# Transposed probabilities in two PSUM banks by turns instead of one, in the first batch's attention

## The chip, the cores and the metric

The kernel runs on one core of a Trainium2 chip, in one launch. The metric is the device time in microseconds, the median of several runs. All tensors are float32.

## What is computed

Three layers follow each other, on a batch of 4 sequences of 768 tokens with 8 heads of 40 channels (320 in all).

1. A recurrence over the tokens with a 40 x 40 state for each head: `state = state * w - (state a) b^T + v k^T`, read by `r`.
2. A mixture of four attention experts, of which the gate picks two for each token. This is the part around the change:

```python
for e in range(E):                       # E = 4 experts, head width 64
    q, k, v = x @ wq[e], x @ wk[e], x @ wv[e]
    scores = np.where(causal, -1e9, scale * (q @ k.transpose(0, 2, 1)))
    a = np.exp(scores - scores.max(-1, keepdims=True))
    a /= a.sum(-1, keepdims=True) + 1e-09
    ye = a @ v @ wo[e]
    out += mask_e * w_e * ye             # gate of the expert for the token
```

3. A gated MLP with 1,024 channels whose second half is normalised and mixed over the tokens by a 768 x 768 matrix (`w_spatial`), multiplied by the first half and projected by `w_out`.

## The kernel before, in words

The recurrence (lines 27 to 1026) takes the first half of the time; its last outputs land in memory, and layers 2 and 3 (`experts_and_mlp`, lines 1027 to 1633) follow batch by batch. Each engine has a program of its own, written out by hand, and they are tied by semaphores: `then_inc` on the producer, `wait_ge` ahead of the consumer. An engine carries out its program in order, so an instruction that waits holds up everything behind it.

TensorE's program for layers 2 and 3 is the loop of lines 1463 to 1484. For batch n it turns the tokens (`turn_x`), multiplies out values, gates, queries and keys, and goes through the attention in 15 steps. Between the steps' parts it issues slices of the *dense* work of batch n-1, that is the mixing over tokens (L1440) and the output projection (L1452). The function `slot` hands them out evenly. Batch 0 has no batch before it, so its attention runs without such slices.

**A step.** The attention of a batch has 12 units (`STEPS`): 6 blocks of 128 queries times 2 pairs of experts. Unit s has block i = s // 2 and pair s % 2, and is causal, so its scores have i + 1 blocks of 128 keys for each of the pair's two experts. At step s TensorE works on three units at once:

- `scores(n, s)` (L1362): scores of unit s into banks 0 to 3;
- `turn(n, m)` (L1382) for each piece m of the step: the probabilities of unit s-2 are transposed, up to four blocks of 128 x 128 at a time, into one PSUM bank, `T_BANK` = 4;
- `times_v(n, s-3)` (L1394): the values times the transposed probabilities of unit s-3, into bank 5.

**Pieces.** The list `pieces` (lines 1114 to 1120) is fixed: unit s-2 has 2 (i' + 1) blocks, for i' its own query block, cut into pieces of four and a last one of two where that is left. In even steps from 4 on a *share* piece of two blocks follows, which transposes each expert's gate over its sum. A batch has 30 pieces. Step by step from 2 to 14 their numbers are 1, 1, 2, 1, 3, 2, 3, 2, 4, 3, 4, 3 and 1.

**The other engines.** VectorE takes the maximum of unit s from the scores' banks and writes the masked scores to `probs` (`maxima`, L1535), makes the shares (L1543 to L1549), and multiplies the product with the values by the transposed share (`scaled_o`, L1557). ScalarE's program in a step alternates (lines 1288 to 1297): copy of the step's first piece out of its bank (`turned`, L1228 is the copying helper), exponential of unit s for the first expert (L1242), copy of the second piece, exponential for the second expert, then the copies of the third and fourth piece.

**Who waits for whom.** `p_turned` counts the transposed pieces and `p_read` the copied ones. Piece m of `turn` waits for `p_read` of piece m-1 (line 1374), since all pieces share bank 4. `times_v` waits for the copies of the pieces of the step before. Behind the 15 steps of batch 0 come `turn_x(1)` and `values_and_gates(1)` (54 transpositions and matmuls), and then `hidden(0)` (L1409), which writes banks 6 and 7 (`M_BANK` = 6 and the next). For batch 0 nothing in layers 2 and 3 uses bank 6 before `hidden(0)`.

The lines that matter:

```python
if n > 0 or m > 0:
    pe.wait_ge(p_read, at(n, p_read, m))           # turn, lines 1373, 1374
...
copy(dst.rearrange("p j t -> p (j t)"), bank[T_BANK][:, 0:k * P]).then_inc(p_read, 1)   # turned, line 1235
```

Of the kernel before, what the change touches and what calls it, by code (L numbers as in the profile page):

```python
# [10 lines left out]
P = 128  # L11
# [1015 lines left out]
def experts_and_mlp(nc, z, x_dram, weights, out_dram, shared):  # L1027
# [15 lines left out]
    ident, hide, before = shared.ident, shared.hide, shared.before  # L1043
    w_qk, w_vg, w_oi, x_tok = shared.w_qk, shared.w_vg, shared.w_oi, shared.x_tok

    with ExitStack() as ctx:
# [5 lines left out]
        def sem(name, count, first=0):  # L1052

            s = shared.stack.enter_context(nc.semaphore(name))
            per[s] = count
            start[s] = first
            return s

        def at(n, s, c):

            return n * per[s] + (c + start[s])
# [26 lines left out]
        out_tok = sb("out_tok", [P, BLOCKS, F])  # L1088


        banks = shared.banks
        bank = [banks[:, i, :] for i in range(8)]
        T_BANK, O_BANK, M_BANK = 4, 5, 6
# [27 lines left out]
        PIECES = len(pieces)  # L1121
        p_turned = sem("p_turned", PIECES)
        p_read = sem("p_read", PIECES)
# [25 lines left out]
        def pieces_of(s):  # L1149

            return [m for m, piece in enumerate(pieces) if piece[0] == s]

        def probs_upto(s):


            return max(m for m, piece in enumerate(pieces) if piece[0] <= s + 2 and piece[1] == "probs") + 1
# [11 lines left out]
        def dense_upto(n, s, k):  # L1168

            return DENSE * (slots.index((s, k)) + 1) // len(slots) if n else 0  # L1170

        def dense_from(n, s, k):

            i = slots.index((s, k))
            return dense_upto(n, *slots[i - 1]) if i else 0

        def groups_of(n, lo, hi):


            ends = [BLOCKS * (g + 1) for g in range(2 * DT)] + [SPATIAL + DT * (g + 1) for g in range(BLOCKS)]  # L1180
            return [g for g, end in enumerate(ends) if lo < end <= hi]
# [11 lines left out]
        def after_recurrence(engine):  # L1193


            for done, count in shared.recurrence_done:
                engine.wait_ge(done, count)
# [27 lines left out]
        @block.scalar  # L1225
        def _(act):
            def copy(dst, src):
                return act.activation(dst, src, ACT.Copy)  # L1228

            def turned(n, m):  # L1230

                s, what, j, k = pieces[m]
                act.wait_ge(p_turned, at(n, p_turned, m + 1))
                dst = probs_t[:, s % 2, j:j + k, :] if what == "probs" else share_t[:, j % 2, :, :]
                copy(dst.rearrange("p j t -> p (j t)"), bank[T_BANK][:, 0:k * P]).then_inc(p_read, 1)

            def exponentials(n, s, a):

                i, e = s // EP, 2 * (s % EP) + a
                width = (i + 1) * P  # L1240
                act.wait_ge(s_read, at(n, s_read, 2 * s + a + 1))
                act.activation(probs[:, s % 3, a, 0:width], probs[:, s % 3, a, 0:width], ACT.Exp, scale=-1.0,  # L1242
                               bias=neg_max[:, i, e:e + 1], accum_out=den[:, i, e:e + 1]).then_inc(probs_ready, 1)

            def outputs(n, lo, hi):

                m = n - 1
                for g in groups_of(n, lo, hi):
                    if n > 0 and g >= 2 * DT:
                        i = g - 2 * DT  # L1250
                        act.wait_ge(y_ready2, at(m, y_ready2, i + 1))
                        if m > 0:
                            act.wait_ge(y_stored, at(m - 1, y_stored, 16 * BLOCKS))
                        copy(out_tok[:, i, :], bank[M_BANK + i % 2][:, 0:F]).then_inc(y_read, 1)

            after_recurrence(act)
            for n in range(B + 1):
                m = n - 1
                if n < B:
                    for i in range(1, BLOCKS, 2):  # L1260
                        act.wait_ge(x_turned, at(n, x_turned, i + 1))
                        t = slice(i * P, i * P + P)
                        src = bank[i % 4]
                        copy(x_t[:, 0:2, t], src[:, 0:2 * P].rearrange("p (k t) -> p k t", k=2))
                        copy(shared.x_last[0:LAST, t], src[0:LAST, 2 * P:3 * P]).then_inc(x_read_act, 1)
                if n > 0:
                    for i in range(BLOCKS):
                        act.wait_ge(h_ready, at(m, h_ready, i + 1))
                        act.activation(v_raw[:, i, :], bank[M_BANK + i % 2][:, :], ACT.Relu,
                                       accum_out=stat[:, 0, i:i + 1]).then_inc(h_read, 1)  # L1270
                    act.wait_ge(mean_ready, at(m, mean_ready, 1))
                    for i in range(BLOCKS):
                        act.activation(v_n[:, i, :], v_raw[:, i, :], ACT.Square, bias=stat[:, 1, i:i + 1],
                                       accum_out=stat[:, 2, i:i + 1]).then_inc(squares_ready, 1)
                if n < B:
                    act.wait_ge(gate_step, at(n, gate_step, 7))
                    act.activation(gate[:, 2, :, :], gate[:, 1, :, :], ACT.Exp).then_inc(gate_exp, 1)
                if n > 0:
                    act.wait_ge(norm_step, at(m, norm_step, 1))
                    act.activation(stat[:, 4, :], stat[:, 3, :], ACT.Sqrt).then_inc(root_ready, 1)  # L1280
                if n < B:
                    for j in range(4):
                        act.wait_ge(qk_ready, at(n, qk_ready, j + 1))
                        act.activation(q_t[:, j // 2, (j % 2) * TH:(j % 2) * TH + TH], bank[j][:, 0:TH],
                                       ACT.Copy, scale=float(HD) ** -0.5).then_inc(q_read, 1)

                    outputs(n, 0, dense_upto(n, -1, 0))
                    for s in range(STEPS + 3):
                        outputs(n, dense_from(n, s, 0), dense_upto(n, s, 0))
                        last = len(pieces_of(s)) + 1  # L1290
                        for k in range(max(2, last)):
                            if k + 1 < last:
                                turned(n, pieces_of(s)[k])
                            if k < 2 and s < STEPS:
                                exponentials(n, s, k)
                            if k + 1 <= last:
                                outputs(n, dense_from(n, s, k + 1), dense_upto(n, s, k + 1))
                else:
                    outputs(n, 0, DENSE)

        @block.tensor
        def _(pe):
# [63 lines left out]
            def turn(n, m):  # L1366

                s, what, j, k = pieces[m]
                if what == "probs":
                    pe.wait_ge(probs_ready, at(n, probs_ready, 2 * (s - 1)))  # L1370
                else:
                    pe.wait_ge(share_ready, at(n, share_ready, j + 1))
                if n > 0 or m > 0:
                    pe.wait_ge(p_read, at(n, p_read, m))
                width = (s - 2) // EP + 1
                for x in range(k):
                    if what == "probs":
                        a, c = (j + x) // width, (j + x) % width
                        src = probs[:, (s - 2) % 3, a, c * P:c * P + P]
                    else:  # L1380
                        src = share_b[:, 2 * x:2 * x + 2, :].rearrange("p e d -> p (e d)")
                    ins = pe.transpose(bank[T_BANK][:, x * P:x * P + P], src, ident[:, :])  # L1382
                ins.then_inc(p_turned, 1)

            def times_v(n, s):
# [13 lines left out]
            def hidden(m):  # L1399

                for i in range(BLOCKS):
                    if i < 2:
                        if m > 0:
                            pe.wait_ge(y_read, at(m - 1, y_read, BLOCKS - 1 + i))
                    else:
                        pe.wait_ge(h_read, at(m, h_read, i - 1))
                    pe.wait_ge(o_read, at(m, o_read, i + 1))
                    for q in range(EP):
                        ins = pe.matmul(bank[M_BANK + i % 2][:, :], o_t[:, q, i * P:i * P + P], w_oi[:, q, DH:],  # L1409
                                        start=(q == 0), stop=(q == EP - 1))  # L1410
                    ins.then_inc(h_ready, 1)
# [362 lines left out]
```

## Time and profile before

| | |
|---|---|
| median of 3 timed runs | 1078.49 us (1078.14 to 1078.82) |
| profiled execution | 1071.31 us, span 1069.5 us |
| mean granted TensorE clock | 0.984 of full speed |
| TensorE busy with matmuls | 989.7 us (93%) |
| VectorE, ScalarE, GpSimd busy | 523.9, 451.9 and 249.2 us |
| first batch's attention | 545.3 to 599.0 us of the span |

The profile shows one execution, and its own time is 7.2 us below the median of the timed runs. Busy times of different engines overlap; for each engine busy time and idle time add up to the span. PE is TensorE's matmuls, PEld its weight loads, DVE is VectorE, ACT is ScalarE. A view of the waits names for each idle time the instruction that ended it. The chain of waits is followed back from the last instruction of the stretch, so its pieces follow each other without overlap.

### The profile page before, as it was taken

Reading aid. Unit: us, or ns where it says so; the run is one execution under the profiler, and the core shown is the slowest. Engines: PE = TensorE matmul, PEld = TensorE weight load, DVE = VectorE, ACT = ScalarE, POOL = GpSimd, SP = SyncE. Lnnn points to the kernel's source line nnn. Section 1 sums busy time; section 2 is a strip of 40 time slices with the busy share of each in tenths; the row PEclk is TensorE's granted clock in tenths of the full one; section 3 lists DMA queues with packets and bytes.
Section 4 is the critical chain, followed back from the end, with each engine's and each line's share of the span. In section 5 each row is a group of like instructions: output and inputs, shape, how many; then the busy total and the mean of one; then the engine's idle time right before and its main releaser. Section 6 shows DMA issues by size and latency. Waiting matters only on the chain.

```text
span 1069.5 us, 36916 instructions
## 1 busy us (share of the span) xinstructions
PE 989.7 (93%) x15696; PEld 708.6 (66%) x15696; DVE 523.9 (49%) x1443; ACT 451.9 (42%) x1116; POOL 249.2 (23%) x352
## 2 busy tenths in 40 slices
PE   1889999999999999998887999999999999999988
PEld 0478888888888888886644654557545665456555
DVE  5357777777777877755343233322433224331220
ACT  1245555655556565553145243442333423434400
POOL 7334454344444534411000001100011000110011
PEclk9869999999999999999999999999999999999989
DMA  5124434334343433221140100001000000000001
GB/s 154 50 67 119 112 110 124 97 100 151 101 124 101 124 95 111 79 70 48 39 164 1 37 1 1 1 19 56 0 1 1 26 13 0 1 1 26 13 0 37
DMA packets 50645, 63.49 MB, mean 59 GB/s; under 512 B 26545, under 2 KB 36593, under 8 KB 50481
## 3 DMA queue, kind: packets, MB, share of 16 engines
q1 hardware_dynamic: 50480, 61.13, 19.6%
q8 instruction: 125, 2.05, 0.8%
q14 instruction: 40, 0.32, 0.1%
HBM read 53.22 MB, written 7.86 MB: 57 GB/s over the span
## 4 chain that ended last, share of the span: by engine, by line
PE 81%; DVE 9%; issue 4%; ACT 3%; POOL 1%; DMA 1%; SPq 1%; DVEq 0%; POOLq 0%; ACTq 0%
PE banks L1440 13%; PE banks L590 10%; PE banks L635 6%; PE banks L1343 6%; PE banks L1382 5%; PE banks L1362 4%; PE banks L1394 4%; PE banks L1422 4%; PE banks L1409 4%; PE banks L1452 4%; PE banks L820 3%; DVE state_z L1016 3%; PE banks L810 3%; PE banks L1329 3%; PE banks L682 2%
## 5 line engine op out<-in xcount | busy, mean ns | idle before, releaser
L473 ACT ACTIVATE powers_z<-powers,parity 128x256 f32<-128x256 f32 x240 | 108.6, 500 | 168.8 <-DVE powers L891 168.8
L1440 PE MATMUL banks<-w_st,v_n 128*128 128x384 f32 x384 | 151.5, 510 | 4.9 <-issue 4.9
L1223 POOL TENSOR_TENSOR v_st<-v_st,u_t 128x384 f32<-128x384 f32 x32 | 31.9, 998 | 513.5 <-DVE v_st L1589 513.5
L635 PE MATMUL banks<-pq,powers_z 64*64 64x64 f32 (+1 forms) x3072 | 135.0, 226 | 6.1 <-ACT pq L465 3.3
L635 PEld LDWEIGHTS banks<-pq,powers_z 64*64 64x64 f32 x3072 | 114.2, 140 | 11.2 <-ACT powers_z L473 4.1
L1228 ACT ACTIVATE probs_t<-banks 128x512 f32<-128x512 f32 (+1 forms) x96 | 52.0, 542 | 145.4 <-PE banks L1382 145.4
L434 POOL TENSOR_TENSOR state<-state_sum,dc 128x160 f32<-128x160 f32 x92 | 68.6, 746 | 177.7 <-DVE state_sum L1002 177.5
L1440 PEld LDWEIGHTS banks<-w_st,v_n 128*128 128x128 f32 x384 | 65.5, 194 | 44.1 <-issue 19.9
L994 DVE SCALAR_TENSOR_TENSOR vu_tok<-banks,minus,vz_tok 128x80 f32<-128x80 f32 x192 | 48.9, 296 | 81.0 <-PE banks L820 80.9
L1535 DVE CUSTOM_DVE_ANT_0 probs<-banks,hide 128x128 f32<-128x128 f32 (+5 forms) x96 | 56.0, 622 | 66.3 <-PE banks L1362 66.1
L1242 ACT ACTIVATE probs<-probs,neg_max 128x128 f32<-128x128 f32 (+5 forms) x96 | 63.2, 660 | 34.5 <-DVE neg_max L1535 34.5
L395 POOL TENSOR_TENSOR kb_ch<-kb_raw,s_ch 128x512 f32<-128x512 f32 x48 | 60.5, 1282 | 52.0 <-issue 33.6
L1382 PEld LDWEIGHTS banks<-ident,probs 128*128 128x128 f32 x336 | 39.1, 141 | 45.9 <-issue 35.0
L1382 PE MATMUL banks<-ident,probs 128*128 128x128 f32 x336 | 54.0, 277 | 13.1 <-ACT probs_t L1228 11.5
L1452 PE MATMUL banks<-w,v_st 128*128 128x320 f32 x192 | 62.1, 443 | 0.0
L1557 DVE TENSOR_TENSOR o_t<-banks,share_t 128x256 f32<-128x256 f32 x24 | 10.2, 425 | 97.4 <-PE banks L1394 96.1
L1589 DVE TENSOR_TENSOR v_st<-banks,bias 128x384 f32<-128x384 f32 x32 | 17.8, 556 | 75.5 <-PE banks L1440 75.3
L601 PE MATMUL banks<-az_ch,kb_ch 128*32 128x64 f32 x1536 | 31.9, 225 | 24.6 <-ACT az_ch L465 23.6
L590 PE MATMUL banks<-ident,state_z 128*128 128x128 f32 x384 | 52.4, 280 | 0.8 <-ACT vu_ch L465 0.8
L1362 PE MATMUL banks<-k_t,q_t 64*128 64x512 f32 (+3 forms) x256 | 48.9, 481 | 1.4 <-DVE k_t L1620 0.7
L1394 PEld LDWEIGHTS banks<-probs_t,vg 128*64 128x64 f32 x672 | 36.6, 139 | 20.5 <-issue 11.3
L1394 PE MATMUL banks<-probs_t,vg 128*64 128x128 f32 x672 | 48.4, 284 | 0.0
(158 smaller groups left out, 1860.1 us busy)
## 6 DMA issues: line engine op xcount, KB each, us to landing
w_ch<-decays_dram SPq DMA_DIRECT2D x48, 160.0 KB
kb_raw<-kb_ch_dram SPq DMA_DIRECT2D x48, 160.0 KB
vz_tok<-vz_tok_dram SPq DMA_DIRECT2D x24, 320.0 KB, 3.5
r_all<-rz_ch_dram SPq DMA_DIRECT2D x48, 160.0 KB
x_dram<-y_tok SPq DMA_DIRECT2D x384, 10.0 KB, 1.9
a_raw<-a_ch_dram SPq DMA_DIRECT2D x48, 80.0 KB
vc_tok<-vc_tok_dram SPq DMA_DIRECT2D x24, 160.0 KB, 3.8
r_all<-r_ch_dram SPq DMA_DIRECT2D x48, 80.0 KB
```

The source lines that it names most:

```text
L395: pool.tensor_tensor(kb_ch[:, u % 3, a * W:a * W + W].rearrange("p (k s t) -> p k s t", s=2, t=C), kb_raw[:, u % 2, a * W:a * W + W].rearr ...
L434: pool.tensor_tensor(state[:, d % 2], state_sum[:, :, :], dc[:, v % 4, d].unsqueeze(2).to_broadcast([P, Q, D]), ALU.mult)\
L473: act.activation(powers_z[:, i, :, j, :], powers[:, i, :, :], ACT.Copy, scale=parity[:, j:j + 1])\
L590: return pe.transpose(to, src, ident[:, :])
L635: ins = pe.matmul(to[r, k * n:k * n + n], powers_z[r, i, k, :, :].rearrange("p j t -> p (j t)"), right, start=True, stop=True)
L1242: act.activation(probs[:, s % 3, a, 0:width], probs[:, s % 3, a, 0:width], ACT.Exp, scale=-1.0, bias=neg_max[:, i, e:e + 1], accum_out=den ...
L1343: ins = pe.matmul(bank[j % 4][:, 0:TH], w_qk[:, which, k, q * P:q * P + P], x_of(k, t), start=(k == 0), stop=(k == NK - 1))
L1362: ins = pe.matmul(bank[2 * a + (j if width > 512 else s % 2)][:, 0:w], q_t[rows, p, i * P:i * P + P], k_t[rows, p, c:c + w], start=True, s ...
L1382: ins = pe.transpose(bank[T_BANK][:, x * P:x * P + P], src, ident[:, :])
L1394: ins = pe.matmul(bank[O_BANK][64 * a:64 * a + HD, p * P:p * P + P], vg[:, j, e * HD:e * HD + HD], probs_t[:, s % 2, a * (i + 1) + j, :], ...
L1440: ins = pe.matmul(bank[M_BANK + j % 2][:, 0:TH], v_n[:, i, d * P:d * P + P], w_st[:, i, t], start=(i == 0), stop=(i == BLOCKS - 1))
L1452: ins = pe.matmul(bank[M_BANK + i % 2][:, 0:F], gated[:, d, i * P:i * P + P], w_2[:, d, :], start=(d == 0), stop=(d == DT - 1))
```

## The change

In batch 0 the pieces with an odd number go to bank 6 (`M_BANK`), those with an even number stay in bank 4. The transposition of piece m there waits for the copy of piece m-2 (the semaphore's value m-1) in place of that of piece m-1, and piece 1 waits for none. ScalarE's copy reads the bank of its piece. The first block of `hidden(0)`, which writes bank 6, waits for the copy of batch 0's last piece. For the batches 1 to 3 all stays as it was.

```diff
+        def turn_bank(n, m):
+            return bank[M_BANK if n == 0 and m % 2 else T_BANK]
...
             def turned(n, m):
...
-                copy(dst.rearrange("p j t -> p (j t)"), bank[T_BANK][:, 0:k * P]).then_inc(p_read, 1)
+                copy(dst.rearrange("p j t -> p (j t)"), turn_bank(n, m)[:, 0:k * P]).then_inc(p_read, 1)
...
             def turn(n, m):
...
-                if n > 0 or m > 0:
+                if n > 0:
                     pe.wait_ge(p_read, at(n, p_read, m))
+                elif m > 1:
+                    pe.wait_ge(p_read, at(0, p_read, m - 1))
...
-                    ins = pe.transpose(bank[T_BANK][:, x * P:x * P + P], src, ident[:, :])
+                    ins = pe.transpose(turn_bank(n, m)[:, x * P:x * P + P], src, ident[:, :])
...
             def hidden(m):
                 for i in range(BLOCKS):
                     if i < 2:
                         if m > 0:
                             pe.wait_ge(y_read, at(m - 1, y_read, BLOCKS - 1 + i))
+                        elif i == 0:
+                            pe.wait_ge(p_read, at(0, p_read, PIECES))
```

## Rows read from the trace of the kernel before

**Rows 1.** The page, busy time, share of the span, instructions.

```profile
PE 989.7 (93%) x15696; PEld 708.6 (66%) x15696; DVE 523.9 (49%) x1443; ACT 451.9 (42%) x1116; POOL 249.2 (23%) x352
```

**Rows 2.** Busy time by stage: length, PE, PEld, DVE, ACT, POOL, PEclk, DMA.

```profile
545.30:599.00 53.70, 39.52 (x329) 25.09 (x329) 20.82 (x72) 29.95 (x78) 0.00 (x0) 0.97 0.04 15
599.00:645.00 46.00, 46.00 (x160) 28.57 (x159) 17.46 (x50) 14.94 (x38) 0.00 (x0) 1.00 0.07 22
```

**Rows 3.** Waits of TensorE, 545.3 to 599: total us, times, longest.

```profile
PE banks L1382 <- ACT probs_t L1228: 13.0, 17, 0.8
```

**Rows 4.** Waits of TensorE, from 599 us to the end.

```profile
PE banks L1440 <- issue: 4.9, 1, 4.9
PE banks L1382 <- ACT probs_t L1228: 2.9, 12, 0.2
```

**Rows 5.** Chain of waits, 538 to 600: start, length, what (steps 10, 11, 12).

```profile
572.34 1.49 PE banks L1362 x8
573.83 0.60 PE banks L1382 x4
574.43 0.02 issue
574.45 0.60 ACT probs_t L1228
575.05 0.91 ACT probs L1242 x2
575.96 0.49 ACT probs_t L1228
576.46 0.91 ACT probs L1242 x2
577.37 0.28 ACT probs_t L1228
577.65 0.14 issue
577.79 0.41 PE banks L1382 x2
578.20 1.02 PE banks L1394 x16
...
583.89 1.24 PE banks L1394 x20
...
589.32 0.66 PE banks L1382 x2
589.97 2.33 PE banks L1394 x20
```

**Rows 6.** Groups of VectorE, 545.3 to 599: busy us, mean ns.

```profile
L1535 DVE CUSTOM_DVE_ANT_0 probs<-banks,hide 128x768 f32<-128x768 f32 x4 | 3.7, 955 | 3.2 <-PE banks L1362 3.2
...
L1535 DVE DVE_READ_ACCUMULATOR2_ANT neg_max<- 128x1 f32 x24 | 2.0, 84 | 0.0
```

**Rows 7.** Transpositions and copies, all batches: ns shortest, median, longest.

```profile
L1382 PE MATMUL banks<-ident,probs x336: 272/273/349, 547.8 to 987.1; 128*128 128x128 f32 x168
...
L1228 ACT ACTIVATE probs_t<-banks x96: 363/597/598, 548.4 to 987.4; 128x512 f32<-128x512 f32 x72, 128x256 f32<-128x256 f32 x24
```

**Rows 8.** Busy time around 588 us, columns as in Rows 2.

```profile
586.00:588.00 2.00, 0.72 (x5) 0.54 (x6) 0.00 (x0) 0.95 (x2) 0.00 (x0) 1.00 0.00 0
588.00:590.00 2.00, 1.22 (x8) 0.68 (x10) 0.00 (x0) 0.60 (x1) 0.00 (x0) 0.73 0.00 0
590.00:592.00 2.00, 2.00 (x20) 1.91 (x20) 0.00 (x0) 0.38 (x1) 0.00 (x0) 0.50 0.00 0
```

**Rows 9.** Busy time at the tail, columns as in Rows 2.

```profile
1018.00:1021.00 3.00, 1.35 (x2) 0.84 (x3) 1.55 (x4) 0.00 (x0) 0.00 (x0) 0.66 0.00 0
1021.00:1024.00 3.00, 3.00 (x6) 1.69 (x5) 0.00 (x0) 0.00 (x0) 0.00 (x0) 0.50 0.00 0
```

## The prediction

> **What bounds the kernel now.** I read the page first, then the busy time by stage, the waits of the stage that the change touches, and the chain of waits through it. On the page TensorE is busy for 93% of the span [rows 1], so a change counts only by what it does to TensorE's idle time or to its clock. By stage that share is uneven: in the 53.70 us from 545.3 to 599.0, which is the first batch's attention, TensorE has work for 39.52 us; in the next 46.00 us it has no idle time at all [rows 2]. This stretch is the only place where the change acts, and it is TensorE's alone: what it wins there moves everything behind it forward, because TensorE is the engine that the rest of the program waits for.
>
> The waits say who is late: 17 times, 13.0 us in all, a transposition stands still for ScalarE's copy of the piece before [rows 3]. That is 0.77 us each, and the number fits the code. A piece waits for the copy of the piece before it whenever nothing stands between them in TensorE's program; steps 4 to 13 have 1, 0, 2, 1, 2, 1, 3, 2, 3 and 2 such neighbours (the share piece of an even step included), together 17. Where a piece is the first of its step, the copy had a product with the values and new scores to hide behind, and no wait shows. In the later batches dense matmuls stand between the pieces, and the same kind of wait costs 2.9 us in 12 times, 0.24 us each [rows 4].
>
> The chain through step 10 shows what one such wait is made of [rows 5]: a piece of four blocks takes 0.60 us, 0.02 us later ScalarE copies it for 0.60 us, and 0.14 us after the copy the next piece starts. It also shows ScalarE's own order: copy, exponential, copy, exponential, copy, with 0.91 us for an exponential with its read and 0.49 us from the start of a four-block copy to that of what follows it. That order decides which waits remain.
>
> **Removed.** All 17 waits are for the bank and not for the data: the exponentials that a piece reads are two steps old. With two banks by turns a piece waits for the copy of the piece before last. Removed: 13.0 us [rows 3].
>
> **New waits.** Each is worked out from the durations of [rows 5], with time 0 at the start of the step's first piece. The copy of that piece ends at 0.60 + 0.02 + 0.60 = 1.22, and its bank can be written at 1.36. If the second piece has four blocks TensorE is through with it at 1.21, and a third piece waits 0.15 us; if it has two blocks (0.41 us), at 1.01, and the third waits 0.35 us.
> - Steps 4, 5, 7 and 9 have at most two pieces: nothing.
> - Step 6 (four blocks, two, share): 0.35. Step 8 (four, four, share): 0.15.
> - Step 10 (four, four, two, share): 0.15 for the third. The fourth needs the second's copy, and before that one ScalarE has an exponential to do, which itself waits for VectorE's maximum: it ends about 0.96 + 0.08 us after the scores [rows 6], so the exponential starts at 1.13, the copy at 2.04, it ends at 2.64, and the bank is free at 2.78. TensorE is ready at 1.36 + 0.41 = 1.77: a wait of 1.01 us, the largest.
> - Step 11 (four, four, two): 0.15. Its third copy comes after both exponentials: 2.04 + 0.50 + 0.91 = 3.45, done at 3.82 (0.37 us, as the shortest copies of [rows 7]). No piece of step 11 waits for it, but the second of step 12 does, from 1.77 + 1.24 (values) + 0.60 = 3.61 until 3.96: 0.35.
> - Step 12's share piece: 0.15. Step 13's third piece: 0.15. Step 14: nothing.
>
> The sum is 0.35 + 0.15 + 0.15 + 1.01 + 0.15 + 0.35 + 0.15 + 0.15 = 2.46 us. The waits removed and the waits added make 13.0 - 2.5 = **10.5 us**. The ends for this term: nothing new at all (13.0 us won), or each of the 8 places above waits a full 0.77 us (13.0 - 6.2 = 6.8 us won). I take the worked value: a late copy is the only cost the rows show, and its parts are each seen here.
>
> **Other terms of the edit.** The new wait at the first hidden product stands behind the last copy, which ends at about the time the last product with the values starts; the next batch's 54 transpositions and first matmuls lie between: nothing, and at most 0.14 us if it were not covered. One wait less for piece 1: nothing, TensorE is not stopped there now. TensorE would now write one bank while ScalarE reads another. That happens already in the later batches, beside the dense matmuls, and over all four batches the copies spread no further than 597 to 598 ns from median to longest and the transpositions' median is 273 ns with a shortest of 272 [rows 7]: I take nothing, the median's case. At worst the 50 transpositions of the 17 pieces take the longest row's 349 ns, 50 x 0.076 = 3.8 us more; a gain is excluded by the shortest. VectorE and the DMA queues get no new instruction. VectorE becomes a little tighter, since scores come sooner: in step 10 its two maxima take about 2 us after the scores, while TensorE has 0.6 + 0.6 + 0.15 + 0.41 + 1.0 + 0.41 + 1.0 us until the next scores, so they are not late.
>
> **The clock.** Between 588 and 592 us the granted clock is 0.73 and then 0.50, that is 1.2 GHz in place of 2.4, right after a stretch in which TensorE had 0.72 us of work in 2.00 [rows 8]. The chain prices it: the twenty matmuls with the values that took 1.24 us in step 11 take 2.33 us in step 12, and the share piece before them 0.66 us in place of 0.41 [rows 5]: 1.09 + 0.25 = 1.34 us. In the new order steps 12 and 13 are filled: TensorE idles 0.65 us in some 7 us. I take it that the clock stays up and add **1.3 us**; the ends are 0 and 1.3. The rule that speaks against this is a section of the Trainium skill, TensorE: Matmul & The Clock Gate, "A second HAM failure mode: psum-queue depth-cycling": a kernel whose matmul groups cycle through PSUM banks leaves many very short idle times, and the clock then oscillates. By that rule the result would be the rival with the low clock below; the trace so far speaks otherwise, since its mean over the stretch is 0.97 [rows 2], and the drop at 588 alone makes that up: (2 x 0.27 + 2 x 0.50) / 53.7 = 0.03. Through all the short idle times before it the clock stayed up. At the tail, the idle time of 4.9 us [rows 4] brings the clock down again (0.66 and 0.50 in six microseconds [rows 9]). All this now lies 12 us earlier and may be longer or shorter: a row of 3 us at low clock is worth 3 x (1 - 1.24 / 2.33) = 1.4 us, which I put into the range on both sides.
>
> **Sum.** 10.5 + 1.3 = 11.8 us. The profiled execution took 1071.31 us (span 1069.5); it would take 1059.5. The median of the timed runs is 1078.49 us, 7.2 us more; no view says where that lies, and I take the gain over unchanged: **1066.7 us**.
>
> **Rivals.**
> - *The clock drop stays* somewhere in the stretch, as short as now: 10.5 us won, 1068.0. For: it has already come once here. Against: the gaps around it go. Chance 0.17.
> - *ScalarE becomes the bound.* It has 29.95 us of work in this stretch [rows 2], and would have it in about 42. If its order (copies behind exponentials) delays the transpositions at every one of the 8 places by 0.77 us, 6.8 us plus some of the clock are won: 1071. For: the 1.01 us of step 10 is such a case. Against: 29.95 is well below 42, and TensorE itself is busy 38 of them (39.52 - 1.34). Chance 0.13.
> - *Low clock over the stretch*, the slower one. If the idle times are now cut so finely that the clock stays at 1.2 GHz, its price is 0.47 us for each microsecond that it lasts (1 - 1.24 / 2.33); 22 us of it eat up the 10.5 us. Over the whole stretch TensorE's 38 us of work would be 72, some 19 us more than the stretch has now: 1098. Against: more work in less time than before. Chance 0.02.
> - *The change does not do what it says*, because the waits are for something else or the time won is waited for again at the next stage: 1078.5. Against: the 17 waits name the copy, and the 46.00 us behind the stretch have no idle time [rows 2]. Chance 0.03.
> - My forecast: 0.65.
>
> **How the numbers follow.** 1066.7 is the likeliest case. The range reaches down by 3.5 us (no new waits would give 2.5, the tail's clock 1.4, and both in full are not likely together) and up by 4.3 to the ScalarE case, which takes in the 3.8 us of slower transpositions and the clock drop at 1068.0 with the tail's 1.4: 1063.2 to 1071.0. A measurement of this kernel can tell about 0.2%, 2.2 us, from no change. Every case but two lies beyond that: faster 0.95, same 0.03, slower 0.02.
>
> **What would show it.** Right: the attention stretch is 41 to 43 us long; the 17 waits for the copy become about 8, with 2.5 us in total and a longest of 1.0 in step 10; the clock is 1.00 all through; TensorE's busy time in the stretch is near 38 us; the next stage still takes 46.0 us. Wrong: ScalarE's copies at 0.60 us grown longer (the two banks do collide), transpositions above 273 ns, waits of TensorE for VectorE's maxima, or a granted clock below 1.00 in the stretch.

## The result, and the profile after

The changed kernel took 1059.75 us (median; the kernel before 1078.14 in the same comparison), a ratio of 0.9862 with a 95% interval of 0.9833 to 0.9891: about 14.9 us less. One of its five executions, the profiled one, took 4513 us, with TensorE busy for 4472.8 us on the same 15,696 matmuls that take 982.5 us in the profile below, and a recorded clock of 1.00; it is left out, why it was slow is open, and the profile below is of another run of the same kernel. Three later comparisons of the unchanged pair gave 0.992 (0.9898 to 0.9941), 0.9877 (0.9845 to 0.9908) and 0.9907 (0.9872 to 0.9942). In microseconds the four are 14.9, 8.6, 13.2 and 10.0, in the mean 11.7, against 11.8 forecast. The forecast's gain holds; its absolute 1066.7 us was 7 us too high, and this median lies below the range as a time, while 0.9862 of 1078.49 is 1063.6, inside it. The forecast was counted from a median of three executions, 1078.49, and the 59 executions of the kernel before that came later, on three chips, have medians of 1071.64, 1069.58 and 1069.98.

The length of the attention stretch is the sharper measure, for it repeats to 0.1 us. I take it from the first scores of batch 0 to the first token transposition of batch 1. The busy time by stage, first of the kernel before (profiled again), then of the changed one (columns: length, PE, PEld, DVE, ACT, POOL, PEclk, DMA share, GB/s):

```profile
30.00:85.00 55.00, 44.20 (x966) 33.36 (x964) 31.36 (x76) 25.02 (x58) 22.89 (x28) 0.94 0.26 79
495.00:546.34 51.34, 43.93 (x550) 32.70 (x551) 17.50 (x52) 8.16 (x21) 2.51 (x4) 0.93 0.32 98
546.34:599.21 52.87, 39.43 (x328) 24.96 (x328) 20.27 (x71) 29.92 (x78) 0.00 (x0) 0.97 0.03 12
599.21:1068.50 469.29, 456.13 (x2092) 267.06 (x2090) 141.51 (x420) 155.62 (x398) 31.90 (x32) 1.00 0.04 13
```

```profile
544.79:585.63 40.84, 36.53 (x329) 24.10 (x329) 19.98 (x71) 29.24 (x78) 0.00 (x0) 1.00 0.04 12
585.63:1055.90 470.27, 457.17 (x2092) 267.58 (x2090) 141.53 (x420) 155.73 (x398) 31.96 (x32) 0.99 0.04 13
```

The stretch fell from 52.87 to 40.84 us, 12.03 less; two more profiles of the changed kernel show 40.83 and 40.82. What lies behind it takes the same time as before to 1 us (469.29 and 470.27), so nothing is given back later. The clock is 1.00 all through the stretch. These answer to [rows 2], whose stretch begins 0.72 us earlier, in the wait for the first keys; counted that way the new stretch is 41.6 us, within the 41 to 43 forecast.

The waits of TensorE in the changed kernel (545 to 600 us: total, times, longest), which answer to [rows 3]:

```profile
PE banks L1389 <- ACT probs_t L1233: 3.6, 8, 1.0
PE banks L1367 <- DVE k_t L1629: 0.7, 1, 0.7
PE banks L1367 <- DVE neg_max L1544: 0.7, 2, 0.4
```

Eight waits for a copy are left of seventeen, as many as forecast, but they are worth 3.6 us and not 2.5. In order of time, TensorE's own rows (start, length, what, and in brackets the idle time before it) show each, in steps 6, 8, 10 (twice), 11, 12 (twice) and 13:

```profile
555.00 0.41 PE L1389 MATMUL banks<-ident,share_b 128*128 128x128 f32 x2 [0.56 <-ACT probs_t L1233]
...
561.67 0.41 PE L1389 MATMUL banks<-ident,share_b 128*128 128x128 f32 x2 [0.34 <-ACT probs_t L1233]
...
567.64 1.09 PE L1389 MATMUL banks<-ident,probs 128*128 128x128 f32 x8
569.07 0.41 PE L1389 MATMUL banks<-ident,probs 128*128 128x128 f32 x2 [0.34 <-ACT probs_t L1233]
570.47 0.41 PE L1389 MATMUL banks<-ident,share_b 128*128 128x128 f32 x2 [0.99 <-ACT probs_t L1233]
...
574.76 0.41 PE L1389 MATMUL banks<-ident,probs 128*128 128x128 f32 x2 [0.34 <-ACT probs_t L1233]
...
576.35 0.66 PE L1389 MATMUL banks<-ident,probs 128*128 128x128 f32 x4
577.36 1.11 PE L1389 MATMUL banks<-ident,probs 128*128 128x128 f32 x8 [0.35 <-ACT probs_t L1233]
578.76 0.41 PE L1389 MATMUL banks<-ident,share_b 128*128 128x128 f32 x2 [0.29 <-ACT probs_t L1233]
...
581.78 0.63 PE L1389 MATMUL banks<-ident,probs 128*128 128x128 f32 x4 [0.34 <-ACT probs_t L1233]
```

Why the sizes are off shows in step 9, of which the chain of waits has this row (start, length, what):

```profile
564.17 1.02 PE banks L1389 x8
```

Two pieces of four blocks with no wait between them take 1.02 us, not 0.60 + 0.61: the second adds only 0.42. TensorE's own rows say where the rest is. Four transpositions with a wait behind them take 0.66 us (at 576.35) and eight in a row 1.09 (at 567.64), so four more cost 0.43, 0.11 each, although one lasts 0.27 us [rows 7]: in a row the next starts while the last still runs. Only ahead of a wait does the last one count in full, 0.16 us more. The 0.60 us of [rows 5] is such a piece; it follows the scores at once and has the wait behind it. Without a wait TensorE is through earlier, and waits longer for a copy that comes when it was expected. In step 10 the third piece starts at 569.07, 1.36 us after the first one's place in the chain, 567.71, exactly as forecast.

### The profile page after: what moved, and what is told of

It reads as the page before. It is cut to its first block, busy times and chain, and to the rows that moved or that the text cites. A ratio compares the mean times of both kernels' runs of the same rounds, so it can differ in the third digit from the quotient of the medians.

```text
span 4511.2 us, 36916 instructions
## 1 busy us (share of the span) xinstructions
PE 4472.8 (99%) x15696; PEld 2804.9 (62%) x15696; DVE 534.9 (12%) x1443; ACT 465.9 (10%) x1116; POOL 241.4 (5%) x352
## 4 chain that ended last, share of the span: by engine, by line
PE 99%; POOL 0%; issue 0%; DVE 0%; ACT 0%; DVEq 0%; POOLq 0%; ACTq 0%
PE banks L635 14%; PE banks L590 13%; PE banks L1449 13%; PE banks L1348 8%; PE banks L1461 5%; PE banks L1389 5%; PE banks L1418 5%; PE banks L1431 5%; PE banks L1367 4%; PE banks L1401 4%; PE banks L1334 4%; PE banks L682 3%; PE banks L601 3%; PE banks L820 3%; PE banks L832 3%; PE banks L804 2%
## 5 line engine op out<-in xcount | busy, mean ns | idle before, releaser
L1449 PE MATMUL banks<-w_st,v_n 128*128 128x384 f32 x384 | 597.3, 1762 | 4.9 <-issue 4.9
L635 PE MATMUL banks<-pq,powers_z 64*64 64x64 f32 (+1 forms) x3072 | 564.9, 654 | 0.5 <-ACT d_tok L465 0.5
L635 PEld LDWEIGHTS banks<-pq,powers_z 64*64 64x64 f32 x3072 | 526.9, 597 | 20.0 <-issue 18.4
L590 PE MATMUL banks<-ident,state_z 128*128 128x128 f32 x384 | 258.2, 1016 | 0.0
L1461 PE MATMUL banks<-w,v_st 128*128 128x320 f32 x192 | 244.1, 1490 | 0.0
L1348 PE MATMUL banks<-x_t,w_qk 128*128 128x384 f32 x128 | 240.7, 2153 | 0.0
L590 PEld LDWEIGHTS banks<-ident,state_z 128*128 128x128 f32 x384 | 171.0, 494 | 61.5 <-issue 60.7
L1418 PE MATMUL banks<-w_oi,o_t 128*128 128x512 f32 x96 | 207.1, 2473 | 0.0
L1431 PE MATMUL banks<-o_t,w_oi 128*128 128x384 f32 x128 | 207.1, 1945 | 0.0
L832 PE MATMUL banks<-vu_tok,kb_tok 64*40 64x40 f32 x1536 | 163.9, 406 | 1.4 <-DVE vu_tok L994 1.4
```

The costliest lines, as they stand in the source:

```text
L590: return pe.transpose(to, src, ident[:, :])
L635: ins = pe.matmul(to[r, k * n:k * n + n], powers_z[r, i, k, :, :].rearrange("p j t -> p (j t)"), right, start=True, stop=True)
L832: ins = pe.matmul(bank[S_BANK + q % 2][rows40(x), a * D:a * D + D], kb_tok[rows64(p), u % 3, a, c, x, :], vu_tok[rows64(p), u % 2, c, a, x ...
L1348: ins = pe.matmul(bank[j % 4][:, 0:TH], w_qk[:, which, k, q * P:q * P + P], x_of(k, t), start=(k == 0), stop=(k == NK - 1))
L1431: ins = pe.matmul(bank[M_BANK + j % 2][:, 0:TH], w_oi[:, q, d * P:d * P + P], o_t[:, q, t], start=(q == 0), stop=(q == EP - 1))
L1449: ins = pe.matmul(bank[M_BANK + j % 2][:, 0:TH], v_n[:, i, d * P:d * P + P], w_st[:, i, t], start=(i == 0), stop=(i == BLOCKS - 1))
```

## The experiments

Each comparison ran against the kernel before on the same chip. All stretch lengths are read as above.

### The kernel before and the changed one again

> The kernel before, unchanged, for its own spread and a second profile. Both theories: ratio 1.000 within 0.003; attention of batch 0 is 53.7 us long (52.3 if the clock does not fall in it), 17 waits of 0.77 us. If the profiled and timed executions differ by several us again, the theory that the low-clock time elsewhere (recurrence start and tail) varies from run to run expects that difference there and not in the attention stretch.

> The changed kernel, unchanged. Theory A (waits and local clock only): 10.5 + 1.3 = 11.8 us less than before in the stretch of batch 0's attention, which lasts 41.9 us with 8 waits of 2.5 us in all, longest 1.0; anything beyond 11.8 us in the medians is granted clock outside the stretch. Rival B (more is won inside the stretch): the stretch is 36 to 38 us long. The measured ratio was 0.9862 (about 15 us); A expects 0.989, B 0.984.

Measured: the kernel before against itself 1.0006 (0.9983 to 1.003), stretch 52.87 us, 17 waits of 13.0 us. Its 12 executions ran from 1065.67 to 1079.54 us, so a single time says little here. The changed kernel: 0.992, stretch 40.84 us. The 41.9 us of theory A were counted from 53.70; from 52.87 the same 11.8 us lead to 41.1. So theory A is right about the stretch to 0.3 us, and rival B, more won inside it, is out.

The spread between executions comes in part with the clock: over the 23 executions of the kernel before in this comparison, time and mean granted clock go together with a correlation of -0.86, and 0.001 less clock goes with 0.7 us more; in the two later comparisons the correlation is -0.65, with 0.6 and 0.5 us. Where that lies shows in the traces: most have low-clock microseconds at 35 to 45 us, at 65 to 80 and at 500 to 515, in the recurrence's start and end, some between 50 and 65 too, and together they make from 7 to 31 us. None of these places is touched by the change.

The recorded clock does not account for all of it. The six traces with 13.7 us of low clock in the recurrence reach the first scores between 540.6 and 546.3 us, and the one with the least, 6.8 us, only at 548.6. In that one, the fourth run of the changed kernel, six matmuls of the recurrence take 5.78 us while the recorded clock is 1.00; in the third run they take 3.04 (start, length, what; the row from 34 to 38 us is busy time by stage):

```profile
31.29 5.78 PE L615 MATMUL banks<-r_all,w_ot 128*128 128x512 f32 x6
...
34.00:38.00 4.00, 4.00 (x36) 1.34 (x34) 0.00 (x0) 0.60 (x1) 0.00 (x0) 1.00 0.19 72
```

```profile
29.06 3.04 PE L615 MATMUL banks<-r_all,w_ot 128*128 128x512 f32 x6
```

So a clock of 1.00 has to be read together with durations. In the attention stretch they agree: TensorE's work there is 36.53, 36.53 and 36.52 us in the three traces.

### The banks without the earlier start

```diff
-                if n > 0:
-                    pe.wait_ge(p_read, at(n, p_read, m))
-                elif m > 1:
-                    pe.wait_ge(p_read, at(0, p_read, m - 1))
+                if n > 0 or m > 0:
+                    pe.wait_ge(p_read, at(n, p_read, m))
```

> Two banks by turns, but each piece waits for the copy of the piece before, as before the change. If the gain is the earlier start alone (theory A): ratio 1.000, stretch 53.7 us with 17 waits of 0.77 us. If writing another bank than the one being read is worth something by itself (rival B): a ratio below 0.997 and shorter waits or transpositions.

Measured: ratio 1.0004 (0.9979 to 1.003), stretch 53.08 us, and the waits of the kernel before:

```profile
PE banks L1387 <- ACT probs_t L1233: 13.0, 17, 0.8
```

The second bank alone is worth nothing (its stretch of 53.08 us is 0.2 us longer than before); all of the gain is the wait that it allows to relax.

### Early and late steps alone

```diff
-                    pe.wait_ge(p_read, at(0, p_read, m - 1))
+                    pe.wait_ge(p_read, at(0, p_read, m - 1 if s < 10 else m))    # early; s >= 10 for late
```

(Piece 1 keeps its wait for piece 0 in the version with the late steps.)

> Two banks, but the wait two pieces back only in steps 2 to 9; from step 10 on each piece waits for the copy just before it. Theory A: the stretch is 52.9 - 4.9 = 48.0 us, with the drop of the clock near its end still there; 10 of the old waits of 0.77 us plus 2 new ones; ratio 0.995. Rival C (ScalarE is late in the next steps and takes the early gain back): the stretch is above 50 us.

> The reverse: each piece waits for the copy just before it in steps 2 to 9, two pieces back from step 10 on. Theory A: the stretch is 52.9 - 5.9 = 47.0 us, less 1.3 us more if the drop of the clock goes with the gaps of steps 12 and 13 (45.7 us in all); 7 waits of 0.77 us and 6 new ones; ratio 0.993. If the clock drop has nothing to do with these gaps it stays and the stretch is 47.0 us.

Measured: late only, ratio 0.9933 (0.99 to 0.9965), stretch 45.73 us, the 45.7 of the case in which the clock drop goes; its clock is 1.00 all through. Early only, ratio 0.9954 (0.9924 to 0.9984), 12 waits of 8.7 us, stretch 49.61 us and not 48.0. The difference is a second clock drop. Of the version with the early steps only, the busy time around the two drops:

```profile
574.00:576.00 2.00, 0.63 (x3) 0.46 (x4) 0.00 (x0) 1.63 (x4) 0.00 (x0) 0.90 0.00 0
576.00:578.00 2.00, 2.00 (x18) 1.61 (x17) 0.00 (x0) 0.38 (x1) 0.00 (x0) 0.50 0.00 0
588.00:590.00 2.00, 1.22 (x13) 1.07 (x14) 0.00 (x0) 0.98 (x2) 0.00 (x0) 0.82 0.00 0
590.00:592.00 2.00, 2.00 (x17) 1.67 (x14) 0.50 (x2) 0.00 (x0) 0.00 (x0) 0.50 0.00 0
```

The first follows the three gaps of step 10. Sixteen matmuls with the values take 1.98 us there where the changed kernel has them in 1.09, eight scores 1.92 in place of 1.56, and the share piece 0.66 in place of 0.41: 1.50 us, and 49.61 less that is 48.1. Both drops lie in the half whose waits were kept, none in the filled half. So each half gives what was counted for it; the ratio of 0.9954 is 4.9 us (1.7 to 8.1), as forecast for one drop, but too wide to tell one drop from two.

### Gaps filled, waits kept

```diff
                 ins.then_inc(p_turned, 1)
+                if n == 0 and s >= 10:
+                    for x in range(2):
+                        pe.transpose(bank[M_BANK][:, x * P:x * P + P], ident[:, :], ident[:, :])
```

This is the kernel before with added work whose result nobody reads.

> The kernel before, with one bank and all its waits, and behind each piece from step 10 on two more transpositions of the identity into bank 6, which nobody reads: TensorE has some work in the gaps, no wait goes. Theory A (the clock falls around 588 us because of these gaps, and that is worth 1.34 us): the clock stays at 1.00 through the stretch; 10 of the additions lie in gaps and cost nothing, 5 do not and cost about 0.2 us each, so the stretch is 52.9 - 1.3 + 1.1 = 52.7 us, ratio 1.000. If the clock falls there for another reason: it falls again and the stretch is 54.0 us, ratio 1.001.

Measured: ratio 1.0012 (0.9984 to 1.004), which by itself tells little; the trace tells it. The stretch, and TensorE's work among the gaps of step 12:

```profile
540.55:593.20 52.65, 41.38 (x358) 27.25 (x358) 20.27 (x71) 29.95 (x78) 0.00 (x0) 1.00 0.03 10
580.00:582.00 2.00, 1.44 (x13) 1.20 (x12) 0.00 (x0) 0.60 (x1) 0.00 (x0) 1.00 0.00 0
582.00:584.00 2.00, 1.16 (x9) 0.71 (x7) 0.00 (x0) 1.06 (x2) 0.00 (x0) 1.00 0.00 0
```

The clock stays at 1.00 with all 17 waits in place (10.8 us in all, since the filler takes part of ten of them), and the stretch is 52.65 us against 52.7 expected. So the clock term is about the gaps, and it can be had without removing the waits, though here the filler costs nearly as much as it saves. That is one trace; the kernel before showed the drop in both of its traces and the version with the banks alone in its one.

### ScalarE's order

```diff
-                            if k + 1 < last:
+                            if k + 1 < last and not (n == 0 and k == 1):
                                 turned(n, pieces_of(s)[k])
+                            if n == 0 and k == 0 and last > 2:
+                                turned(n, pieces_of(s)[1])
```

> Two banks as in the change, and in batch 0 ScalarE copies the first two pieces of a step before its two exponentials. Theory A (the wait of 0.99 us in step 10 is the exponential between the two copies): it shrinks to 0.2 to 0.4 us, the others stay, stretch 40.1 us (0.7 less), ratio 0.988. Rival (the wait is ScalarE's total work): the wait moves to the next step and the stretch stays at 40.8 us.

Measured: ratio 0.988 (0.9833 to 0.9927), stretch 39.77 us, 1.07 less than the changed kernel. In step 10 the third piece keeps its wait and the fourth has none:

```profile
572.67 0.41 PE L1391 MATMUL banks<-ident,probs 128*128 128x128 f32 x2 [0.34 <-ACT probs_t L1233]
573.16 0.41 PE L1391 MATMUL banks<-ident,share_b 128*128 128x128 f32 x2
```

The largest remaining wait was the exponential between two copies, as the forecast had it. It was expected to shrink to 0.2 to 0.4 us, for 0.7 us won; it is gone whole, 0.99 us, and TensorE's work is 0.07 us shorter with it. ScalarE carries out the same instructions as before, so their total was not the bound.

### Three banks

```diff
-            return bank[M_BANK if n == 0 and m % 2 else T_BANK]
+            return bank[(T_BANK, M_BANK, M_BANK + 1)[m % 3] if n == 0 else T_BANK]
...
-                elif m > 1:
-                    pe.wait_ge(p_read, at(0, p_read, m - 1))
+                elif m > 2:
+                    pe.wait_ge(p_read, at(0, p_read, m - 2))
```

> Three banks by turns (4, 6, 7) in batch 0, each piece waits for the copy three pieces back. Theory A: nearly all of the 2.5 us of waits left by two banks go, with one of about 0.2 us for VectorE's maxima before the scores of step 8; the stretch is 39.5 us, 2.3 us less than with two banks, ratio 0.987 or lower. If ScalarE's order is the bound (rival C): not more than 0.5 us less than two banks.

Measured: ratio 0.9895 (0.9869 to 0.9921), stretch 37.92 us, 2.92 less than with two banks, where 2.3 were expected: rival C is out. The waits that are left are mostly of another kind (0.38 us of the first row, ahead of the second scores, was there before the change):

```profile
PE banks L1367 <- DVE neg_max L1544: 1.0, 3, 0.4
PE banks L1401 <- DVE o_t L1566: 0.6, 1, 0.6
PE banks L1389 <- ACT probs_t L1233: 0.6, 1, 0.6
```

VectorE is late, and its own row says for whom: it stood still 2.27 us for the share's copy, which ScalarE does behind both exponentials of step 6, and what VectorE has queued behind that product are the maxima that the scores of step 8 wait for:

```profile
556.69 0.43 DVE L1566 TENSOR_TENSOR o_t<-banks,share_t 128x256 f32<-128x256 f32 x1 [2.27 <-ACT share_t L1233]
557.03 0.68 DVE L1544 CUSTOM_DVE_ANT_0 probs<-banks,hide 128x512 f32<-128x512 f32 x1
```

So the last version also puts ScalarE's copies first, and all of them:

```diff
+                            if n == 0:
+                                for piece in (pieces_of(s) if k == 0 else []):
+                                    turned(n, piece)
-                            if k + 1 < last:
+                            elif k + 1 < last:
                                 turned(n, pieces_of(s)[k])
```

> Three banks by turns and, in batch 0, all of a step's copies ahead of its exponentials on ScalarE. With three banks TensorE still waits 0.63 us for VectorE's scaled output, 0.34 and 0.29 for its maxima and 0.56 for a copy, and VectorE is late in steps 6 and 7 because the copy of the share stands behind two exponentials. Theory A: the waits for VectorE in steps 7 and 8 go, the stretch is 36.6 us (37.9 with three banks alone, 40.8 with two), ratio 0.985. Rival: exponentials that start later hold up the transpositions two steps on, and the stretch is 38 us or more.

> The changed kernel on the chip of these two runs, to stand beside the version with three banks: stretch 40.8 us, ratio 0.989 (the interval of the earlier ones holds 0.988 to 0.992).

Measured: three banks with the copies first 0.9839 (0.9804 to 0.9874), stretch 36.20 us; the changed kernel beside it 0.9907, stretch 40.82.

```profile
543.29:579.49 36.20, 35.20 (x329) 24.22 (x329) 20.27 (x71) 28.79 (x78) 0.00 (x0) 1.00 0.04 15
```

TensorE has work for 35.20 of the 36.20 us, and one wait for a copy, 0.5 us, is left beside 0.38 us ahead of the second scores. This version beats both kernels: 16.7 us less than the kernel before by the stretch.

### The changed kernel a third time

> The changed kernel once more, because two comparisons with the kernel before gave 0.986 and 0.992. Theory A (about 12 us won in the attention stretch, the rest is which low-clock stretches an execution happens to get in the recurrence): ratio between 0.986 and 0.992, near 0.989; the stretch from the first scores to the next batch's first token transposition again 40.8 us. Rival B (the gain differs from chip to chip in the stretch itself): another length of the stretch.

Measured: 0.9877 (0.9845 to 0.9908), stretch 40.83 us, on another chip. The ratios differ by 4 us and the stretch does not. Theory A.

## Why the prediction was right

**The bound.** Right. TensorE's idle time in the stretch was the whole prize, and the stages behind it moved forward by it.

**Removed waits.** Right in number and cause: 17 waits, all for the bank; the version with banks alone keeps all.

**New waits.** The eight places are those forecast. Their sizes, forecast then measured: step 6 0.35 and 0.56; step 8 0.15 and 0.34; step 10 0.15 and 0.34, and 1.01 and 0.99; step 11 0.15 and 0.34; step 12 0.35 and 0.35, 0.15 and 0.29; step 13 0.15 and 0.34. The term of 2.46 us was 3.55. What was off is the step "if the second piece has four blocks TensorE is through with it at 1.21": it costs 0.42 us, not 0.61, when it follows the first at once. The durations of [rows 5] were those of pieces next to a wait. Of the 0.19 us, 0.16 is the last transposition of the first piece, which runs to its end there and is overlapped in a row; the rest, 0.03, is the start behind a wait.

**That error appears twice, with opposite signs.** The waits came out 1.1 us longer, and TensorE's busy time shorter by more than the clock: from 39.43 to 36.53 us, 2.90, where the clock gives 1.34 and 1.56 is left. The forecast had 38. The balance in the stretch, by differences of the rows: waits for copies 13.0 - 3.6 = 9.4; busy time 2.9; waits for VectorE's maxima 0.4 before and 0.7 after, -0.3; together 12.0, and 12.03 measured. The forecast's 10.5 + 1.3 was right in sum, and for most of it that is not luck. In steps 6, 8, 10, 11, 12 and 13 a later piece still waits for a copy, which comes at the same time either way: the time that TensorE saves becomes wait (six times 0.14 to 0.21 us, the 1.1 us above). Only in steps 4, 7 and 9, where no wait is left, is it won, some 0.5 us that the sum had left out; and 0.3 us of that went to the wait for VectorE, which it had left out as well. That these two nearly cancel is luck.

**VectorE.** "They are not late" held for step 10, the one that was worked out, and failed for step 7, which was not. In the chain of waits of the changed kernel there is a piece that had no counterpart before (start, length, what):

```profile
556.53 0.28 ACT share_t L1233
...
557.61 0.68 DVE probs L1544
558.29 0.01 DVE neg_max L1544
558.30 0.60 DVE probs L1544
558.90 0.02 DVE neg_max L1544
558.92 0.04 issue
558.96 1.35 PE banks L1367 x8
```

The scores of step 8 wait for VectorE, which waited for the share's copy. It costs 0.30 us here. With three banks the waits for VectorE are the larger part of what is new or left: 0.63, 0.34 and 0.29 us against 0.56 for a copy.

**The clock.** Right, and borne out by three experiments: the drop is gone in all three traces of the changed kernel, gone in the one trace with the late half alone and in the one with filled gaps, and the one trace with the early half alone has two drops. The rule of the Trainium skill that spoke against the change (TensorE: Matmul & The Clock Gate, "A second HAM failure mode: psum-queue depth-cycling") did not come true here: with the wait relaxed in all steps the clock stayed at 1.00 through the stretch in all six traces, three of the changed kernel, one with copies first and two with three banks. The drops followed the waits of one piece for the next, not the cycling through banks: the version with the banks alone cycles as the changed kernel does, keeps the waits, and has the drop (0.74 and 0.50 between 586 and 590 us).

**ScalarE, and bank against bank.** ScalarE's order set the one large wait, its total did not matter. Writing one bank while ScalarE reads another cost nothing: the transpositions of all batches have 272, 273 and 332 ns as shortest, median and longest where [rows 7] had up to 349, and the copies of probabilities a median of 597 and a longest of 603, against 597 and 598.

**The level.** Only the absolute time was off, by the median it started from.

## What to carry to other kernels

Where a buffer is reused at once, count its waits by where neighbours stand in the waiting engine's program, then work out for each whether the second buffer hides the reader's time plus the reader's own queue: the order of the reader's other work decides what is left, and putting the copies ahead of work that is needed later was worth another 1 us here. A duration taken from a group that ends ahead of a wait holds the whole of its last instruction; where the next group follows at once, that end is overlapped. When single executions spread by 10 us, measure the stretch that the change touches in the trace, and take ratios from many executions, not from three.

## What was not expected

- Two groups of four transpositions back to back take 1.02 us, one ahead of a wait 0.60 to 0.63 us: every wait removed on TensorE saved 0.17 us of busy time beyond its own length (1.56 us for 9 fewer waits), most of which the waits that stayed gave back.
- Gaps of the same length bring the clock down in one execution and not in the other. After the three gaps of step 10 it fell in the version with the early steps only (0.63 us of work in the two microseconds before 576), and in both traces of the kernel before, with the same gaps (0.62 and 0.55 us of work between 576 and 578), it stayed up there and fell after those of step 12. What decides between them stays open.
- The recurrence, which the change does not touch, ends up to 8 us earlier or later from one trace to another, two thirds of what this change won. Its recorded low clock, 7 to 31 us, does not order them: the first scores start at 548.6 us in the trace with the least of it and at 548.9 and 548.5 in the two with the most. Slow matmuls at a recorded clock of 1.00 are part of the difference; what brings them is open.
